# Attention, routed experts and a dense layer in one kernel: first tiles, queues and weight splits rearranged

## Time and profile before

| | us |
|---|---|
| median of three runs | 1018.84 (1018.44 to 1019.17) |
| the profiled execution | 1019.02 |
| its span in the profile | 1017.3 |
| busy: TensorE matmul | 990.1 |
| busy: VectorE | 411.2 |
| busy: ACT | 231.5 |
| busy: POOL | 423.3 |

### The profile page before, as it was taken

One profiled execution on the slowest core, in us unless ns is written; L12 is line 12 of the kernel. 1 busy time (PEld: TensorE's weight loads), 2 busy tenths in 40 slices (PEclk: granted clock), 3 DMA queues, 4 the chain that ended last, 5 costly groups with the idle time before them and its releaser, 6 DMA issues.

```text
span 1017.3 us, 18019 instructions
## 1 busy us (share of the span) xinstructions
PE 990.1 (97%) x7108; PEld 878.8 (86%) x7108; DVE 411.2 (40%) x889; ACT 231.5 (23%) x545; POOL 423.3 (42%) x326
## 2 busy tenths in 40 slices
PE   7989879999999999999999999999999999999998
PEld 6767668889889898989989989999999999999997
DVE  3567854312222222213222255545445445355333
ACT  4767611111111111111111121111111211111111
POOL 3158977992845739192855729101001001000000
PEclk9999979999999999999999999999999999999999
DMA  9599877763453717163442433200101111000000
GB/s 184 124 211 245 270 256 247 244 205 111 140 181 95 226 63 206 71 186 115 125 145 90 148 105 124 64 32 21 42 31 41 42 30 41 31 1 1 32 1 31
DMA packets 125879, 115.94 MB, mean 114 GB/s; under 512 B 64913, under 2 KB 93521, under 8 KB 125809
## 3 DMA queue, kind: packets, MB, share of 16 engines
q1 hardware_dynamic: 106368, 75.36, 27.4%
q10 hardware_dynamic: 13680, 20.75, 6.2%
q0 software_dynamic: 5760, 18.88, 5.7%
HBM read 75.90 MB, written 39.06 MB: 113 GB/s over the span
## 4 chain that ended last, share of the span: by engine, by line
PE 88%; POOL 4%; DMA 3%; SPq 1%; DVE 1%; issue 1%; ACT 1%; ACTq 0%; POOLq 0%
PE PS L1647 21%; PE PS L1630 21%; PE PS L1767 20%; PE PS L1751 19%; PE PS L1614 2%; POOL x_sorted L715 1%; POOL W L694 1%; PE PS L1434 1%; PE PS L1510 1%; POOL W L684 1%; PE PS L1692 1%; PE PS L1473 1%; PE PS L1489 1%; DMA k_later<-in_k_dram 1%; SPq L504 1%
## 5 line engine op out<-in xcount | busy, mean ns | idle before, releaser
L1647 PE MATMUL PS<-W,hs_room 128*128 128x512 f32 (+1 forms) x960 | 245.0, 398 | 0.2 <-DVE hs_room L1215 0.2
L1630 PEld LDWEIGHTS PS<-xs,W 128*128 128x128 f32 x1536 | 230.8, 189 | 10.7 <-issue 0.2
L1630 PE MATMUL PS<-xs,W 128*128 128x256 f32 (+2 forms) x1536 | 239.9, 306 | 0.0
L1767 PE MATMUL PS<-W,gs 128*128 128x512 f32 x864 | 217.0, 395 | 0.9 <-DVE gs L1365 0.9
L1751 PE MATMUL PS<-x2s,W 128*128 128x384 f32 x1152 | 216.6, 337 | 0.0
L1751 PEld LDWEIGHTS PS<-x2s,W 128*128 128x128 f32 x1152 | 201.2, 188 | 7.2
L684 POOL TENSOR_TENSOR W<-stage,ones_f 128x1024 fp32r<-128x1024 f32 (+1 forms) x100 | 147.7, 1486 | 138.5 <-PE PS L1647 135.7
L1647 PEld LDWEIGHTS PS<-W,hs_room 128*128 128x128 f32 (+1 forms) x960 | 172.1, 186 | 34.9 <-DVE hs_room L1215 0.4
L1767 PEld LDWEIGHTS PS<-W,gs 128*128 128x128 f32 x864 | 161.2, 188 | 31.8 <-issue 1.6
L694 POOL TENSOR_TENSOR W<-stage,W 128x1024 fp32r<-128x1024 f32 (+1 forms) x100 | 185.6, 1864 | 5.9
L1215 DVE SCALAR_TENSOR_TENSOR hs_room<-PS,hs_room 128x256 fp32r<-128x256 f32 (+2 forms) x128 | 61.9, 484 | 291.7 <-ACT hs_room L911 291.7
(11 more groups left out here) (134 smaller groups left out, 576.5 us busy)
## 6 DMA issues: line engine op xcount, KB each, us to landing
stage<-in_moe_w_dram SPq DMA_DIRECT2D x64, 512.0 KB, 4.6
x_sorted<-zeros SPq DMA_DIRECT2D x7, 1280.0 KB, 7.6
y_sorted<-y_sb ACTq DMA_DIRECT2D x33, 256.0 KB, 3.3
x_in<-x_sorted ACTq DMA_DIRECT2D x31, 256.0 KB, 4.1
vD<-in_v_dram SPq DMA_DIRECT2D x72, 64.0 KB, 3.7
out_dram<-o_sb SPq DMA_DIRECT2D x18, 256.0 KB, 2.1
stage<-in_moe_w_in_dram SPq DMA_DIRECT2D x8, 512.0 KB, 4.0
stage<-in_moe_w_out_dram SPq DMA_DIRECT2D x8, 512.0 KB, 3.6
```

Of the source, the lines that this page charges most:

```text
L1630: last = nc.tensor.matmul(HP_[:, c % 2, 0:n], W[:, par, 0, b, at:at + P], xs[part][:, a, kd, 0:n], start=start, stop=(kd == KD - 1 and (a, ...
L1647: last = nc.tensor.matmul(Y[0:n, first + t, :], hs[:, c % 2, a, t * P:t * P + n], W[:, par, 1, b, c * DM:(c + 1) * DM], start=(c == 0 and ...
L1767: last = nc.tensor.matmul(OP[:, tt, :], gs[:, c % 2, a, tt * P:(tt + 1) * P], W[:, 1, c // FC, b, at:at + DM], start=(c == 0 and (a, b) == ...
```

## The change

- Chunk 0 of q and k is loaded and turned by tile (all eight heads of tile r, `turn_tile`) instead of by head half; scores(0) need tile 0 alone. Each of the two items goes to its own pair of banks, TensorE makes scores(0) between the two, and VectorE takes the row maxima of tile 0 ahead of its copy of tile 1. Item 2 goes to the two banks of the output product and waits for no exps.
- Chunks of q and k in which no batch ends (4 and 8) have four transfers instead of six; the semaphore is raised by the missing 32.
- v(0) is issued by ACT, in two blocks, around its first copy; the two gate weights are issued by POOL and have their own semaphore. Both leave the SP queue.
- On POOL the weight splits before lot 2's scatters go from five to three (`SPLIT_AT`), the scatters end at T = 14 instead of 15, chunk 3 instead of chunk 5 is split between the scatters of lot 2, each scatter now ahead of its piece, with two copies of x_new among them. Chunks 4 and 5 are split behind. Chunks 6 and 7 (`BESIDE`) are split by ACT (high part) and VectorE (low part) in expert 0, after hidden blocks 2 and 3.
- On SP the last of expert 0's weight chunks is loaded after the first rows, and of expert 1's chunks only two (instead of four) ahead of the last zeros of y and the padding.

The diff, cut to its core ("..." marks what is left out):

```diff
-    FIRST_AT = (4, 6, 8, 10, 12, 13, 14, 15)
-    SPLIT_AT = (7, 8, 11, 12, 13)
+    FIRST_AT = (4, 6, 8, 10, 12, 13, 14)
+    SPLIT_AT = (7, 8, 11)
+    BESIDE = 2
...
-    SCATTER_AT = {8: 0, 9: 1, 10: 2, 12: 3, 13: 4, 14: 5, 15: 6}
+    SCATTER_AT = {8: (0,), 9: (1,), 10: (2,), 12: (3,), 13: (4, 5), 14: (6,)}
...
-                if c and c % 2 == 0 and r == (crossed or [0])[0]:
+                if r in crossed(c):
...
+        def item_bank(n, side):
+            return PS[:, 5 + side, :] if n == 2 else SC[:, item_buf(n), side, :]
...
-            return 2 if T < 2 else min(T + AHEAD - 1, ITEMS)
+            return T + 1 if T < 2 else min(T + AHEAD - 1, ITEMS)
...
+        def load_v_block(eng, t, s):
+            b, i = half(t, s)
+            for x in range(2):
+                eng.dma_start(vD[WIN * x:WIN * (x + 1), t % RV, s, :, 0:D],
+                              v[b].rearrange("(h x) r d -> x r h d", x=2)[x, i * WIN:(i + 1) * WIN])\
+                    .then_inc(v_full[t % RV], 16)
...
+                if c % 2 == 0 and not crossed(c):
+                    sp.sem_inc(raw_full[raw_slot(c)], 32)
...
             load_qk(1, both)
             load_qk(2, both)
-            load_v(0)
+            load_v(1)
             load_qk(3, both)
-            load_v(1)
-            for n, w in enumerate((wg, wn)):
-                sp.dma_start(wgn[:, :, n * E:(n + 1) * E], ...).then_inc(s_small, 16)
             load_v(2)
...
             for j in range(PARTS[0][1]):
                 sp.wait_ge(x_loaded[j], 16)
-            load_expert(1, 0, QCH)
+            load_first(SCH - 1)
+            load_expert(1, 0, QCH - BESIDE)
             for n in range(len(ZERO_AT), ZERO_PARTS):
                 zero_y(n)
...
-            load_expert(1, QCH)
+            load_expert(1, QCH - BESIDE)
...
+            for n, w in enumerate((wg, wn)):
+                nc.gpsimd.dma_start(wgn[:, :, n * E:(n + 1) * E], ...).then_inc(s_gates, 16)
             pool.wait_ge(m_all, 5)
...
-                if T in SCATTER_AT:
-                    scatter(SCATTER_AT[T], 0)
+                transfers = [(t, k) for t in SCATTER_AT.get(T, ()) for k in range(2)]
+                if transfers:
+                    scatter(*transfers[0])
                 if T in SPLIT_AT:
                     first_there(SPLIT_AT.index(T))
                     split_hi(0, SPLIT_AT.index(T), PIECES)
-                elif T in SCATTER_AT:
-                    pause()
-                if T in SCATTER_AT:
-                    scatter(SCATTER_AT[T], 1)
+                for t, k in transfers[1:]:
+                    if T not in SPLIT_AT:
+                        pause()
+                    scatter(t, k)
...
-            for n in range(2 * PIECES):
+            for n in range(2 * LOTS[FIRST_LOT][1]):
+                scatter(LOTS[FIRST_LOT][0] + n // 2, n % 2)
                 if n < PIECES:
                     split_hi(0, c, PIECES, n, n + 1)
                 else:
                     split_lo(0, c, c + 1, PIECES, n - PIECES, n - PIECES + 1)
-                scatter(LOTS[FIRST_LOT][0] + n // 2, n % 2)
-            for c in range(len(SPLIT_AT) + 1, SCH):
+                if n % 4 == 3:
+                    keep_x(kept)
+                    kept += 1
...
+            for c in range(len(SPLIT_AT) + 1, SCH - BESIDE):
...
+            pool.sem_inc(w_half, BESIDE)
...
             nc.scalar.preload_act_table_set("natural_log_exp_and_others")
+            load_v_block(act, 0, 0)
             move_first(0)
+            load_v_block(act, 0, 1)
             move_first(1)
             exps(0)
+            move_pt(0, 0)
             move_first(2)
...
+            def beside_hi(c):
+                act.wait_ge(stage_full[c % STAGES], 16 * (c // STAGES + 1))
+                at = slice((c - QCH) * CH, (c - QCH + 1) * CH)
+                nc.scalar.copy(W[:, 0, 1, 0, at], stage[:, c % STAGES, :]).then_inc(beside_half, 1)
...
+                    if first and c in (2, 3):
+                        beside_hi(SCH - BESIDE + c - 2)
...
             move_second(0)
+            row_max(0)
             move_second(1)
-            row_max(0)
             row_max(1)
...
+            def beside_lo(c):
+                at = slice((c - QCH) * CH, (c - QCH + 1) * CH)
+                dve.wait_ge(w_ready, c)
+                dve.wait_ge(beside_half, c - (SCH - BESIDE) + 1)
+                nc.vector.tensor_tensor(W[:, 0, 1, 1, at], stage[:, c % STAGES, :], ...,
+                                        ALU.subtract).then_inc(w_ready, 1)
...
                     h_lo(e, 0, c)
+                    if first and c == 3:
+                        for n in range(SCH - BESIDE, SCH):
+                            beside_lo(n)
...
+            def turn_tile(r):
+                pe.wait_ge(raw_first[r], 64)
+                for side in range(2):
+                    for h in range(HP):
+                        last = nc.tensor.transpose(SC[:, r, side, h * P:(h + 1) * P], ..., ident[:])
+                last.then_inc(ld_full, 1)
...
-            turn_qk(0)
-            turn_qk(1)
+            turn_tile(0)
             scores(0)
+            turn_tile(1)
             scores(1)
+            transpose_p(0, 0)
             turn_qk(2)
-            transpose_p(0, 0)
             turn_qk(AHEAD)
             transpose_p(0, 1)
```

More of the change, by code:

```diff
@@ L376, in half, with crossed @@
             return divmod(2 * T + s, KB)
+        def crossed(c):
+            return [r for r in range(TK) if half(c * TK + r, 0)[0] != half(c * TK + r, 1)[0]]
         def pieces(c):
[L381 to L382 removed]
+            assert len(crossed(c)) <= 1 and not (crossed(c) and c % 2)
             for r in range(TK):
[L384 removed]
+                if r in crossed(c):
                     for s in range(2):
```

68 lines of the change are left out of this document (32 added, 36 removed).

## The result

The changed kernel took 1016.34 us in the median of ten runs (1013.35 to 1018.45) beside 1018.6 for the kernel before: ratio 0.9975 [0.9965, 0.9985], a gain of 2.3 us. Two more comparisons of the same kernel gave 0.9965 [0.9952, 0.9978] and 0.9967 [0.9957, 0.9978], 3.1 us each. Forecast were 5.8 us. The profiled execution took 1013.78 us (span 1011.8), near the lowest of its ten: the three quickest of them (1013.35, 1013.78, 1014.53) have a mean granted clock of 0.995, the other seven (1015.03 to 1018.45) 0.990 to 0.992.

A forecast was written before the change was run, and what follows sets the result against it. The SP queue was taken to pace the attention up to 60 us, the POOL queue its end. SP 5.0 + POOL 0.5 + VectorE 0.3 = 5.8 us off 1018.84 gave 1013.0 us; 8 in 10 range 1009.4 to 1015.9.

The forecast's parts named there:

- The start: Tiles 0 and 1 of the attention: scores(0) near 7.9 us, scores(2) near 17.2; TensorE 3.3 us sooner, between 1.5 and 4.
- The gain of the start is eaten by this wait: At chunk 5: a wait of about 2 us stays, so TensorE goes on 5.0 us sooner, not 8.4.
- The SP queue up to chunk 5: SP's issues in the attention: 3.1 + 2.0 + 0.5 - 0.6 = 5.0 us sooner, between 3.9 and 6.4.
- I take 0.6: SP queue: cost of v(0)'s 256 KB on ACT's queue ahead of SP's bytes, 0.6 us, between nothing and 1.25.
- The wait at chunk 5: TensorE's wait for q and k of chunk 5: about 2 us stays, with the low clock behind it.
- rival A: SP queue lets go: chunk 5's wait shrinks to tenths, clock need not fall; 8.9 us at most, 1009.9; chance 0.27.
- Behind chunk 5: Attention after chunk 5: SP keeps its 5.0 us, TensorE as far behind it as before.
- The POOL queue: Before lot 2's scatters: 10 us of work off POOL buy 0.5 us, as the slots set the start.
- VectorE's routing may be quicker: With less of POOL beside it, VectorE's routing gains 0.3 us, between 0 and 1.
- x_in and the stretch to the end: Wait for x_in about 3.6 us; from expert 0's first hidden block on, the same 878 us as before.
- rival D: Slower: the last chunk's load comes late in expert 0, delaying VectorE's part of hidden block 4; 1021 us; chance 0.03.
- Rival B: Gain paid back at the end, something else holding the first rows: 2 to 4.5 us stay, 1015.5; chance 0.17.

The follow-up runs named there:

- the 18 matmuls ahead of x_in: Changed kernel plus 18 matmuls on zeros (128x128) ahead of TensorE's wait for the first rows of x_in: 1010.74 us (0.993), repeated 1011.03 us (0.9932).
- the disturbed set: Kernels before, changed, v(0) back on SP, no start's part, each with 18 zero matmuls before x_in: 1030.36, 1021.73, 1023.77, 1021.86 us; plain kernel before 1031.05.

## Why the prediction was wrong

The sign was right, the size was not: 2.3 to 3.1 us measured, 5.8 forecast, and the first median lies 0.4 us above the range (1015.9); the two later ones, 1015.21 and 1015.03, lie inside it, but with a shift of the first hidden matmul that is 1.7 to 2.4 us short of the forecast in all three profiles.

- **The start**: scores(0) came 0.6 us and scores(2) 0.3 us sooner than forecast. "The gain of the start is eaten by this wait", meant of chunk 5, failed. It is eaten 35 us sooner, at chunk 2, whose landing the text never held against the earlier TensorE. The turn of chunk 2 stood before at 22.03 and did not wait for its bytes; after, it is there at 20.9, 21.3 and 20.8, and at 21.0 without the start's part, but at 19.1 with v(0) left on SP. So v(0) on ACT, charged with 0.6 us of SP's queue alone, also cost chunk 2 some 2 us. With the half clock behind that wait, which is new, scores(3) to (6) come 0.4 to 0.8 us later than before.
- **The SP queue up to chunk 5**: "its place at 13.54 is taken by v(1) with the same hold-up (4.59 us)" and "I take 0.6" were mis-sized. v(0) on ACT sets SP's first v back by 1.8 us, not 0.6. Chunk 5 comes 4.5, 3.6 and 2.7 us sooner in the three profiles of the changed kernel, and with v(0) left on SP 2.2. So the move brought 1.4 us (the mean 3.6 less 2.2, against a single profile), where 2.5 (3.1 less 0.6) had been booked; the 2.5 left for the gate weights and chunk 4 measured 2.2. The rule of the Trainium skill (DMA: Bandwidth & Descriptors, Issuing engines are not separate DMA queues) pointed the right way: the 1.25 us that the forecast worked out for it were nearer than the 0.6 taken, and still too few here.
- **The wait at chunk 5**: a remaining 2 us were forecast; it was 0, 0 and 0.8 us in the three profiles, since TensorE came later than forecast. With it the half clock of 60 to 66 us went, 1.7 us, which the forecast had kept and rival A had named. So scores(9) came out right (5.2, 4.9, 4.3 us sooner, forecast 5.0) by luck: the start brought nothing and SP less than forecast, and the wait and the clock were given back.
- **Behind chunk 5**: "After it SP keeps its 5.0 us, and TensorE is as far behind it as before" is the step that failed and cost the most: of the 5.0 us only 3.0, 2.6 and 2.0 are left at scores(16). SP's lead falls to 1.0 us at chunk 8; k of chunk 7 is issued in 4.74 us where it took 3.23. Where before TensorE waited for no chunk behind 5, waits of 1.3, 1.8 and 1.2 us in all come back at chunks 6 and 7. With v(3) off SP scores(16) stand at 5.0 us sooner (102.45), chunk 8 is issued 2.5 us sooner than before, and the first hidden matmul is 6.6 sooner: so in that profile it was SP's queue that held the attention there. The two transfers that chunk 8 saves did not make up for it. Why the issues last longer is not shown; from 46 to 95 us the core's queues move 214 GB/s before and 213 after, which fits a queue held by bytes; but v(3) on ACT moved the same bytes, and SP came sooner.
- **The POOL queue**: the mechanism was right, one term too small. POOL was idle 7.0 us (6 forecast), and 0.9 us lay between slot_cur and the scatter (0.3 forecast). But "VectorE's routing may be quicker; 0.3 us, between 0 and 1" measured 1.2 us. From scores(16) to the first hidden matmul POOL's part brought 1.1, 1.3 and 1.4 us where 0.8 (0.5 + 0.3) were forecast, so the loss in the attention is larger than the sum shows.
- **x_in and the stretch to the end**: the wait was 4.46, 4.26 and 4.05 us (3.6 forecast), and the stretch behind it, forecast at the same 878 us, took 876.8, 877.6 and 878.1.
- **VectorE, the last two chunks** (rival D): no sign of it, nothing in the first 12 us of expert 0 but busy time on TensorE.

Sum by profiles: first hidden matmul 4.1, 3.9 and 3.4 us sooner, not 5.8. Of these the attention brought 3.0, 2.6 and 2.0 (5.0 forecast). The medians gained 2.3, 3.1 and 3.1. The remaining us or so is put down to spread: runs of the changed kernel lie 5 us apart, and a half clock of 3 us, worth some 1.6, comes in some executions at 118 or 120 us and in others not, and behind x_in it ends at 134 in one profile and at 138 to 140 in the others. In the first ten runs the mean granted clock goes with the time (0.995 in the three quickest, 0.990 to 0.992 in the rest, some 3 to 5 us over the span); in the later two sets of the same kernel it does so weakly or not at all (1013.04 us at 0.991, 1017.52 at 0.992). So the clock is part of the spread, not all of it.

Rival B's size (1015.5) was nearest, but not its mechanism: nothing held the first rows at the end, the lead was gone before.

The best of all versions is the changed kernel with the 18 matmuls ahead of x_in: 1010.74 and 1011.03 us, 7.6 and 7.1 us below the kernel before, over twice what the change itself brought. It depends on where TensorE stands: in the disturbed set the same matmuls brought the kernel before nothing.

## What to carry to other kernels

When a queue is relieved, follow the new instant to the next transfer that the faster engine will want, and the one after, before booking it: here the first check (chunk 2) and the last ones (chunks 6 to 8) were left out, and each took part of the gain. A lead on a queue whose issues are held is not kept. Ask of an engine that is relieved which other engine works quicker beside it: POOL's idle time gave VectorE 1.2 us just where the slots were made. And look at what a wait costs beyond itself: behind 4 us without matmuls TensorE ran at half clock for some 10 us, which filling the gap took away at no other cost, more than the reordering of three queues had brought.

## What the runs showed of the hardware

- Two queues that issue together slow each other's issues: with v(0)'s four transfers on ACT, SP's first v came 1.8 us later in the mean of eight profiles each, though ACT's own issues took 2.7 us in all, and chunk 2 was there at 20.8 to 21.3 us in place of 19.1.
- VectorE's small instructions take longer beside a busy POOL: 0.67 us against 0.19 for the same one, and 5.81 to 6.04 us against 4.60 to 4.64 for the way from scores(16) to slot_cur (4 and 16 profiles).
- Matmuls on zeros keep the granted clock at 1.00 (2.4 GHz) across a wait. After the 18 (4.18 us) a further 2.77 us of idle time in the kernel before did not lower it either.
- The half clock that follows a wait has no fixed length between executions: behind x_in it lasted 6.8, 10.2 and 10.2 us in three profiles of the changed kernel, and the first hidden matmuls took 2.24, 3.52 and 4.03 us.
- One chip gave 1031 us for the kernel before in one comparison and 1018 in the next; the mean granted clock was 0.9866 and 0.9914, some 5 of the 13 us, and the profiles show more waits between engines and short stops between instructions.
